# Identity transposes ahead of the first scores, an earlier start for the first MLP, and earlier splitting of its weights

## The reference

```python
# q, k, v: (4, 8, 576, 64); x: 2304 tokens x 512; weights 512x2048 and 2048x512
scores = q @ k.T / 8
thresh = max(scores, axis=-1) - tau
scores = where(scores >= thresh, scores, -1e9)
attn   = exp(scores - max); attn /= sum(attn) + 1e-9
x      = (attn @ v) laid out as 2304 tokens x 512
h = x @ w_in;  g = h * sigmoid(1.702 h);         x = g @ w_out      # first MLP
h = x @ w_in2; g = h * tanh(log(1 + exp(h)));    out = g @ w_out2   # second MLP
```

## Time and profile before

| | us |
|---|---|
| median of three executions | 1164.55 |
| profiled execution, its own time | 1164.05 |
| its span (first to last instruction) | 1162.3 |
| PE busy in the span | 1118.1 (96%) |
| DVE busy | 759.1 (65%) |
| ACT busy | 724.1 (62%) |
| POOL busy | 295.4 (25%) |

### The profile page before, as it was taken

How to read it: one execution, slowest core, us unless ns; L and a number is a source line. 1 busy time by engine, 2 the same in 40 slices (tenths; PEclk the granted TensorE clock), 3 DMA queues, 4 the chain that set the end, 5 groups by cost and what they waited for, 6 DMA issues and landing times.

```text
span 1162.3 us, 19359 instructions
## 1 busy us (share of the span) xinstructions
PE 1118.1 (96%) x7472; PEld 1035.4 (89%) x7472; DVE 759.1 (65%) x1359; ACT 724.1 (62%) x995; POOL 295.4 (25%) x502
## 2 busy tenths in 40 slices
PE   8978889999999999999999999999999999999998
PEld 4568889998999999999999999998999989899997
DVE  4678788888888888888888434665433444344343
ACT  3678787767777777777767322467545554554453
POOL 3557674434444433344333000000000000000000
PEclk9989999999999999999999999999999999999999
DMA  2443534232143222233231003520010000000000
GB/s 65 140 131 114 158 86 111 59 94 85 48 111 91 64 82 77 79 105 83 70 103 28 26 19 106 190 76 28 6 49 1 28 28 28 28 28 28 1 28 27
DMA packets 92923, 78.71 MB, mean 68 GB/s; under 512 B 47520, under 2 KB 78752, under 8 KB 92832
## 3 DMA queue, kind: packets, MB, share of 16 engines
q1 hardware_dynamic: 92832, 77.49, 22.9%
HBM read 63.83 MB, written 13.63 MB: 67 GB/s over the span
## 4 chain that ended last, share of the span: by engine, by line
PE 78%; DVE 11%; ACT 7%; issue 3%; POOL 0%; DMA 0%; SPq 0%; ACTq 0%; DVEq 0%
PE ps_s L743 17%; PE ps_r L628 14%; PE ps_r L648 11%; PE ps_r L766 9%; PE ps_t L492 6%; PE ps_t L513 5%; PE ps_t L766 4%; PE ps_s L477 4%; PE ps_t L648 3%; PE ps_r L513 2%; PE ps_s L466 2%; DVE x_pair L585 2%; DVE pt_lo L574 2%; ACT pv_half_sb L544 1%; DVE neg_max L554 1%
## 5 line engine op out<-in xcount | busy, mean ns | idle before, releaser
L628 PE MATMUL ps_r<-x_hi,wi_lo 128*128 128x256 f32 x544 | 158.5, 291 | 2.7 <-DVE x_lo L701 2.7
L810 DVE COPY hidden<-ps_s 128x768 f32<-128x768 f32 x48 | 45.8, 956 | 170.5 <-PE ps_s L743 170.5
L628 PE MATMUL ps_r<-x_lo,wi_hi 128*128 128x256 f32 x544 | 154.2, 284 | 0.0
L628 PE MATMUL ps_r<-x_hi,wi_hi 128*128 128x256 f32 x544 | 154.2, 283 | 0.0
L492 PE MATMUL ps_t<-ident,e_buf 128*128 128x128 f32 x720 | 118.1, 283 | 27.1 <-DVE pt_lo L574 14.5
L839 ACT ACTIVATE m_lo_raw<-m_lo_raw 128x1536 f32<-128x1536 f32 x24 | 35.8, 1491 | 168.8 <-DVE m_lo_raw L817 168.8
L561 DVE SCALAR_TENSOR_TENSOR e_buf<-ps_s,neg_thr,e_buf 128x576 f32<-128x576 f32 x144 | 117.0, 813 | 29.4 <-ACT e_buf L521 22.9
L648 PE MATMUL ps_r<-g_hi,wo_lo 128*128 128x256 f32 x464 | 135.4, 292 | 0.0
L537 ACT CAST pt_hi<-ps_t 128x640 fp32r<-128x640 f32 x128 | 89.0, 695 | 71.8 <-PE ps_t L492 69.6
L743 PE MATMUL ps_s<-x_hi,wi_lo 128*128 128x384 f32 x384 | 129.0, 336 | 2.4 <-DVE x_lo L799 2.4
L492 PEld LDWEIGHTS ps_t<-ident,e_buf 128*128 128x128 f32 x720 | 84.7, 143 | 52.1 <-issue 29.2
(11 more groups left out here) (105 smaller groups left out, 3009.9 us busy)
## 6 DMA issues: line engine op xcount, KB each, us to landing
k_ll_raw<-in_k SPq DMA_DIRECT2D x56, 288.0 KB, 2.9
v_st_raw<-in_v SPq DMA_DIRECT2D x64, 160.0 KB, 2.9
wi_lo_raw<-in_moe_w_in SPq DMA_DIRECT2D x16, 512.0 KB, 3.8
wo_lo_raw<-in_moe_w_out SPq DMA_DIRECT2D x16, 512.0 KB, 4.8
q_raw<-in_q SPq DMA_DIRECT2D x32, 192.0 KB, 2.9
x_scratch<-y_acc SPq DMA_DIRECT2D x9, 512.0 KB, 3.2
x_lo_raw<-x_scratch SPq DMA_DIRECT2D x6, 768.0 KB, 4.7
out_rows<-rows_out SPq DMA_DIRECT2D x18, 256.0 KB, 2.1
```

Source lines behind the costliest of these rows:

```text
L628: mm = pe.matmul(bank[:, part * CH:(part + 1) * CH], wi[w][:, k, f * P:(f + 1) * P], x[:, k, :], start=t == 0, stop=t == 3 * KT - 1)
```

## The change

- PE runs 12 transposes of the identity into an unused part of a PSUM bank ahead of the first scores, and three more behind the scores at each n from 0 to 3.
- `READY[0]` is 18: the first half of chunk 0's MLP is placed at step 18, and the 32 halves are spread over steps 18 to 42. From step 43 on the placement is the same.
- At step 18 ACT copies the last group's x out and rounds it ahead of `act_p_hi` of step 16; DVE takes the remainder of this last x in step 18, ahead of its `dve_p_lo`.
- The slots of the weights move ahead: 4, 6, 8, 10, 12, 14, 16, 18, 21, 23, 26, 28, 30, 31, 34, 35 in place of 9, 12, 14, 17, 19, 21, 23, 24, 26, 28, 30, 31, 33, 34, 36, 37. DVE takes the remainders of seven chunks in place of four. SP issues each load three steps ahead of its slot in place of four.

```diff
-READY = [GROUPS[g][4] + (4 if c == 0 else 8) for c, g in enumerate(CHUNK_GROUP)]
+READY = [GROUPS[g][4] + (3 if c == 0 else 8) for c, g in enumerate(CHUNK_GROUP)]
-        W_SLOT = dict(zip((9, 12, 14, 17, 19, 21, 23, 24, 26, 28, 30, 31, 33, 34, 36, 37), W_ORDER))
+        W_SLOT = dict(zip((4, 6, 8, 10, 12, 14, 16, 18, 21, 23, 26, 28, 30, 31, 34, 35), W_ORDER))
-        W_FIRST = 4
+        W_FIRST = 7
+        def pe_idle(pe, count):
+            for _ in range(count):
+                pe.transpose(ps_r[:, 1, 384:512], ident[:, :], ident[:, :])
...
             pe.wait_ge(s["ident_ready"], 1)
+            pe_idle(pe, 12)
             pe_scores(pe, 0)
...
                         pe_pv(pe, GROUP_AT[n - 3])
+                    if n < 4:
+                        pe_idle(pe, 3)
                     continue
...                                                     # ACT
-                    if n >= 2:
+                    if 2 <= n < FRONT + 2:
                         act_p_hi(act, n - 2)
...
                     if n in X_HI_FIRST:
                         act_x_hi_first(act, X_HI_FIRST[n])
+                    if n == FRONT + 2:
+                        act_p_hi(act, n - 2)
...                                                     # DVE
-                if n - 1 in X_HI_FIRST:
-                    dve_x_lo_first(dve, X_HI_FIRST[n - 1])
+                for late in (1, 0):
+                    if n - late in X_HI_FIRST and (X_HI_FIRST[n - late] < KT - 1) == (late == 1):
+                        dve_x_lo_first(dve, X_HI_FIRST[n - late])
...                                                     # SP
-                if n + 4 in W_SLOT:
-                    w_load(sp, 0, W_SLOT[n + 4])
+                if n + 3 in W_SLOT:
+                    w_load(sp, 0, W_SLOT[n + 3])
```

## The result

The changed kernel takes 1166.58 us (median of 20 executions, 1164.98 to 1172.95) against 1164.32 us (20 executions of the kernel before beside them, 1163.68 to 1165.31). The ratio is 1.0024, 95% interval 1.0018 to 1.0030: slower by 2.3 us, where I forecast 6.4 us faster. Its profiled execution took 1166.24 us, with a span of 1164.4.

A forecast was written before the change was run, and what follows sets the result against it. PE was taken to bound the kernel, the first 187 us deciding through PE's idle time and a low clock to about 25 us. Terms 5.0 - 3.5 + 1.9 + 3.0 = 6.4 us: 1164.55 to 1158.2 us, range 1154.5 to 1167.

The forecast's parts named there:

- Term 1: Opening: identity transposes bring TensorE's clock up early; 5.0 us gained, bounds -2.55 to +5.8.
- The walk of the opening: Masks at 8.3, 10.9, 13.6, 16.3, scores of step 5 at 17.2; first product with v ends at 20.7, not 25.7.
- If it rises: Opening: if the clock rises, the loop of minimum, exponential and mask binds, and 5.0 us are gained.
- rival (a): Opening: the transposes don't lift the clock; -2.55 us there, 1165.7 us in all; chance 0.25.
- rival (b): Opening: the clock rises late or falls back, so half of Term 1; 1162 us in all; chance 0.13.
- low bound of -2.55: Opening with the clock low: transposes cost 0.3 us at the start, then 3 x 0.75 at n = 1, 2, 3.
- Term 2: Weights' roundings at slots 4, 6, 8, 10: four new PE gaps of 0.87 us, -3.5 us; bounds 0 to -5.6.
- Rival (c): Plain part: gaps in even steps thin PE, so the clock falls, about 3 us each; 1169 us; chance 0.12.
- Term 3: Steps 16 to 21: first half starts at 73.5, not 77.53, second clock fall gone; +1.9 us, bounds 0 to +4.
- Term 4: Steps 21 to 43: one half less and eight roundings where eleven were; +3.0 us, bounds +0.5 to +5.
- The fewer roundings: Steps 21 to 43: eight roundings for eleven, 3.1 us less for ACT; taken as 2.0 of PE's 11.7 us idle.
- The half less: Steps 21 to 43: one MLP half less to do there, at most 1.44 us; taken at 1.0.

The follow-up runs named there:

- e5: Kernel before plus identity transposes: 12 ahead of the first scores, 12, 6, 6, 6 behind the scores at n = 0 to 3; 1160.50 us, ratio 0.9962.
- e1: Kernel before plus the change's identity transposes alone (12 ahead, three behind the scores at n = 0 to 3); median 1165.49 us, two executions at 1158.2 and 1158.4.
- e4: Changed kernel without any identity transposes; 1164.89 us, ratio 1.0015 to the kernel before.
- e2: Kernel before with the new weights' slots, seven chunks' remainders on DVE and shorter load distance alone; 1165.89 us, ratio 1.0035.
- e6: Changed kernel without transposes, first eight weights' slots one step later, at odd steps 5 to 19; 1158.69 us, ratio 0.9953 to the kernel before.
- e3: Kernel before with the halves starting at step 18, last x rounded ahead of step 16's copy, its remainder in step 18; 1162.52 us, ratio 0.9984.
- e9: Kernel before plus the 12 transposes ahead of the first scores, none behind later scores; 1164.07 us, ratio 0.9998.
- e11: Kernel before with step 18's orders alone (last x rounded ahead of step 16's copy, remainder in step 18), first half still at step 19; 1161.05 us, ratio 0.9976.
- e10: Changed kernel with 12, 6, 6, 6 transposes in place of 3, 3, 3, 3 behind the scores at n = 0 to 3; 1163.20 us, ratio 0.9983 to the kernel before.
- e8: Kernel before with the edits of e5 and e3 together, weights as before; 1156.36 us, ratio 0.9941.
- e12: Kernel before with e5's transposes, odd weights' slots 5 to 19 and step 18's orders, first half at step 19; 1152.90 us, ratio 0.9906.
- e7: Changed kernel with the transposes of e5 and the odd weights' slots of e6; 1154.75 us, ratio 0.9927 to the kernel before.

## Why the prediction was wrong

**Term 1, the transposes (+5.0), is the step that failed.** The walk of the opening at full clock was right to 0.1 us: e5's first product ends at 20.6 (20.7 walked), its mask 5 is 5.10 early. What failed is the step "If it rises": I took +5.0 on the rise and its lasting, and neither came. In twelve of the twenty executions, those around the median, the clock by their mean grant never rose in the opening: that is rival (a), at 0.25, with 1165.7 forecast and 1166.2 to 1167.4 measured. e1 has the term alone, -1.4 us in the medians and -1.6 in the profiled execution. In the profiled execution of the changed kernel and five or six more it rose and fell back: rival (b), at 0.13, whose 1162 put the term half way between +5.0 and -2.55 (its 3.8 is half of 7.55, not of 5.0); it measured -1.0 at the end of the first product, for each three slow transposes took 0.7 us. The low bound of -2.55 held. That the clock can fall in the opening could have been read before: both falls in the earlier trace rows follow stretches in which PE is thin, and by my own walk PE has, between the end of the first eight score matmuls and the first mask (8.3), only three transposes of 0.44 us. In the changed kernel that stretch was busy 1.36 of 2.5 us. Why twelve transposes raise the clock in some executions only, no run shows.

**Term 2, the roundings (-3.5), was right**: four gaps of 0.85, 0.95, 0.85, 0.95. What I left in a rival is that the thinner PE loses the clock: once in this part of the profiled execution (1.7 us), twice in that of e4. Rival (c) had the mechanism; its price of about 3 us a fall was near (3.3 in e4), and by their times it is the two executions at 1171.7 and 1173.0, not the median. That the thinness is the cause is argued from e4 and e2 against e6, whose roundings leave no gaps and whose five executions show no such time.

**Term 3, steps 16 to 21 (+1.9), was too small:** 3.5 us from mask 14 to mask 20. The first half was walked to 73.5; less the 6.36 us by which the changed kernel was late there it came at 71.8 (78.16 - 6.36), so slot 16's rounding, which I had let delay the product by 1.04, did not show (masks 16 to 17: -0.56 us here, -0.57 in e3 and e9 without a rounding there; each is without the fall that the kernel before has at 62.5). e11 has the cause of the gain: the remainder no longer behind the weight's, and no slow half. How much is the order and how much the fall that stays away was not separated.

**Term 4, steps 21 to 43 (+3.0), was 2.0 too large.** 0.85 of it is the third fall, at 134.8 us (from the comparison with e10), which the prediction's rivals had only for the plain part. The fewer roundings gave 1.8 (e2) where I took 2.0. The half less, taken at +1.0, gave nothing: e10, with the same placement and no fall there, gets 1.85 back from mask 20 to 43, e2 with the old one 1.78. I had counted halves, and not looked at which steps receive two; without a fall it costs 0.2 to 0.6 us in the other kernels (e8 against e5, e3 against e11, e6 against e12).

**The sum by its terms**, for the profiled execution: -1.0 - 3.6 - 1.7 + 3.5 + 1.0 = -1.8 where 6.4 was forecast; 6.0 of the 8.2 are term 1. In the executions whose clock never rose, term 1 is -1.6 by e1 and the rest can't be split up without a profile.

## What to carry to other kernels

Filler work that may raise TensorE's clock is a chance and not a gain: look at every execution's mean grant before you trust the one that was profiled. And a rise is soon lost where the next stretch is thin: count PE's busy time from there to where steady work begins, at full clock, and fill the waits, not only the start. A long operation on an in-order engine costs by what stands behind it: the same four roundings cost 4.5 us or 0.9 by one step's shift. And before two profiles are set against each other, see that the same falls of the clock are in both: here one fall of 1.35 us made a spread of work that costs 0.2 to 0.6 us look as if it cost 2.0.

## What was not expected of the hardware

A run of identity transposes can raise the granted clock: at 4.46 us in e12, with nothing else on PE before the first scores at 4.31, and at 5.1 to 5.2 in the changed kernel, e5 and e8. In none of the six profiles without transposes does it rise before 24 us. But with the same twelve transposes it stays low to the first product in e1 and e9, and to 16 us in e7 and e10, whose opening is that of e12. So executions of one kernel differ in where the clock changes: e1 has 1158.2 and 1166.2, e2 1165.3 and 1173.5, while the kernel before stays within 1163.5 to 1165.4 in 35. Why the early rise comes in some executions and not in others, I leave open: no run sets it apart.
